# Carried attention blocks made whole, two address alignments in TensorE's program, and weight blocks split after the second network's input

## The reference

```python
# attention: q, k, v, f_logit are (4, 8, 768, 48)
f = 1 / (1 + exp(-f_logit))
for t in range(S):
    state = f[:, :, t, :, None] * state + einsum('bhd,bhe->bhde', k[:, :, t], v[:, :, t])
    y[:, :, t] = einsum('bhd,bhde->bhe', q[:, :, t], state)
x = y as (3072, 384)
# first network, d_ff = 1536
xn = x / sqrt(mean(x * x) + 1e-6) * rms_g
x = (silu(xn @ w_gate) * (xn @ w_val)) @ w_out
# second network, d_ff = 2048
h = x @ w_in
g = where(h >= 1, h, where(h <= -1, 0, (h + 1) ** 2 / 4))
out = g @ w_out
```

## Time and profile before

| | |
|---|---|
| median of 3 runs | 938.35 us (938.14 to 938.43) |
| profiled execution | 938.0 us |
| its span, first to last instruction | 936.2 us |
| granted TensorE clock | 1.000 |
| TensorE matmuls busy | 924.3 us, 99% of the span |
| TensorE weight loads busy | 784.0 us, 84% |
| VectorE busy | 555.2 us, 59% |
| ScalarE busy | 329.1 us, 35% |
| GpSimd busy | 15.7 us, 2% |

### The profile page before, as it was taken

One profiled execution on the slowest core, in us unless ns is written; L12 is line 12 of the kernel. 1 busy time (PEld: TensorE's weight loads), 2 busy tenths in 40 slices (PEclk: granted clock), 3 DMA queues, 4 the chain that ended last, 5 costly groups with the idle time before them and its releaser, 6 DMA issues.

```text
span 936.2 us, 18634 instructions
## 1 busy us (share of the span) xinstructions
PE 924.3 (99%) x7498; PEld 784.0 (84%) x7498; DVE 555.2 (59%) x971; ACT 329.1 (35%) x561; POOL 15.7 (2%) x35
## 2 busy tenths in 40 slices
PE   7999999999999999999999999999999999999998
PEld 4999999998888888888888788888888888888886
DVE  7987667756746675576545555445445445555453
ACT  4653233323223232332243433343334333333433
POOL 1000000000000000000000000000000000000000
PEclk9999999999999999999999999999999999999999
DMA  9622533532432341343222100000000000000000
GB/s 317 234 69 62 161 97 98 178 89 86 124 93 74 112 143 55 100 119 108 73 72 86 58 1 0 1 34 0 2 32 0 34 0 0 34 0 0 34 1 34
DMA packets 52129, 65.84 MB, mean 70 GB/s; under 512 B 14560, under 2 KB 42976, under 8 KB 52064
## 3 DMA queue, kind: packets, MB, share of 16 engines
q1 hardware_dynamic: 51920, 64.75, 22.1%
q10 hardware_dynamic: 144, 0.13, 0.0%
HBM read 51.43 MB, written 13.43 MB: 69 GB/s over the span
## 4 chain that ended last, share of the span: by engine, by line
PE 97%; issue 2%; DVE 1%; POOL 0%; ACT 0%; POOLq 0%; DVEq 0%; ACTq 0%
PE gate_ps L599 16%; PE val_ps L599 16%; PE acc L675 14%; PE gate_ps L663 10%; PE acc L621 10%; PE val_ps L663 10%; PE acc L679 7%; PE acc L625 5%; PE pair_ps L462 2%; PE y_ps L485 2%; PE y_ps L525 2%; PE pair_ps L514 1%; PE acc L690 0%; DVE low L1369 0%; PE pair_ps L445 0%
## 5 line engine op out<-in xcount | busy, mean ns | idle before, releaser
L950 ACT ACTIVATE raw<-raw,columns 128x512 f32<-128x512 f32 x96 | 69.4, 723 | 156.6 <-DVE raw L1392 156.6
L675 PE MATMUL acc<-high 128*128 128x512 f32 x282 | 109.9, 390 | 0.0
L675 PE MATMUL acc<-high,low 128*128 128x512 f32 x282 | 109.9, 390 | 0.0
L621 PE MATMUL acc<-high 128*128 128x512 f32 (+2 forms) x252 | 90.1, 362 | 0.0
L621 PE MATMUL acc<-high,low 128*128 128x512 f32 (+2 forms) x252 | 89.4, 359 | 0.0
L957 ACT ACTIVATE high<-qd 128x512 fp32r<-128x512 f32 x96 | 60.7, 632 | 73.1 <-DVE qd L1397 73.1
L679 PE MATMUL acc<-low,high 128*128 128x512 f32 x282 | 79.2, 389 | 0.0
L1392 DVE TENSOR_SCALAR raw<-val_ps 128x512 f32<-128x512 f32 x48 | 33.2, 691 | 77.5 <-PE val_ps L663 77.5
L1392 DVE TENSOR_SCALAR raw<-gate_ps 128x512 f32<-128x512 f32 x48 | 33.1, 689 | 62.7 <-PE gate_ps L663 62.7
L1329 DVE TENSOR_TENSOR low<-qd,high 128x512 fp32r<-128x512 f32 x96 | 65.7, 685 | 5.7 <-ACT high L957 5.1
L599 PE MATMUL gate_ps<-high 128*128 128x512 f32 (+2 forms) x252 | 66.3, 371 | 1.5 <-issue 0.6
(11 more groups left out here) (142 smaller groups left out, 1696.2 us busy)
## 6 DMA issues: line engine op xcount, KB each, us to landing
raw<-qkf_dram SPq DMA_DIRECT2D x22, 770.0 KB, 4.7
x_all<-wb_dram SPq DMA_DIRECT2D x12, 576.0 KB, 5.3
kd_turn_dram<-after SPq DMA_DIRECT2D x19, 256.0 KB, 3.0
kd<-kd_turn_dram SPq DMA_DIRECT2D x76, 64.0 KB, 2.5
v_sb<-v_dram SPq DMA_DIRECT2D x23, 192.0 KB, 2.9
v_early<-v_dram SPq DMA_DIRECT2D x23, 192.0 KB, 3.0
out_dram<-x_all SPq DMA_DIRECT2D x5, 768.0 KB, 3.8
x_turn_dram<-x_all SPq DMA_DIRECT2D x19, 192.0 KB, 1.8
```

The source lines that it names most:

```text
L621: pe.matmul(acc[:, m, 0:width(i)], wb_part(w, j, 2, m), h_hi[:, j % 2, 0:width(i)], start=(j == 0 and w is w_hi), stop=False)
L675: pe.matmul(acc[:, m, 0:N2], wc_part(w, j, 1, m), h2_hi[:, j % 2, :], start=(j == 0 and w is w_hi), stop=False)
L950: nc.scalar.activation(act2_buf[:, j % 2, :], act2_buf[:, j % 2, :], ACT.Square, bias=half_col[:, :], scale=0.5).then_inc(square_ready, 1)
```

## The change

Three things are edited.

The table `APART` and the parameter `state_done` go. Every carried block is issued whole, at its slot.

Two address alignments are put into TensorE's program, ahead of `project_out(1, 4)` and `project_out(3, 7)`.
In the last tile of the first network, VectorE's half of splitting weight blocks 13 and 14, which stood after j = 11, moves behind the low part of the second network's last input columns (line 1383) and of the last h, ahead of block 15. The edit is in VectorE's `gated_mlp`; ScalarE's order stays as it is.

```diff
-APART = {(2, 1): 2, (3, 0): 2, (3, 2): 2, (4, 0): 2, (5, 0): 2, (6, 1): 2}
+LINE = 256
+BEGINS = {(1, 5): 207, (3, 8): 254}
...
-                def attend(n, c, scores_next=False, state_done=False):
+                def attend(n, c, scores_next=False):
...
-                    if not state_done:
-                        attend_state(n, c)
+                    attend_state(n, c)
...
                 def attend_tile(i, slot, blocks):
                     for c, due in enumerate(blocks):
-                        sooner = APART.get((i, c), 0)
-                        if sooner and slot == due - sooner:
-                            attend_state(begin(i) + c, c)
                         if slot == due:
-                            attend(begin(i) + c, c, scores_next=c + 1 < len(blocks), state_done=sooner > 0)
+                            attend(begin(i) + c, c, scores_next=c + 1 < len(blocks))
...
                         value(i, j)
                         if following is not None:
                             attention(following, 3 * j + 1)
+                        if (i, j) in BEGINS:
+                            pe.addr_align(LINE, BEGINS[i, j])
                         if j > 0:
                             project_out(i, j - 1)
...
                         elif j == 1:
                             split_x2(0)
-                        else:
+                        elif j < JB - 1:
                             for jc in wc_due(j):
                                 split_wc(jc)
                     if following is None:
                         split_x2_last()
                     rest_h(i, JB - 1)
                     if following is None:
-                        for jc in wc_due(JB):
+                        for jc in (*wc_due(JB - 1), *wc_due(JB)):
                             split_wc(jc)
```

## The result

The changed kernel took 940.54 us (median of 12 executions, 938.85 to 942.22), the kernel before, run beside it, 938.24 us (12 executions, 937.54 to 940.41). The ratio is 1.0023, with a 95% interval of 1.0016 to 1.0030. That is slower by 0.23%, just above the 0.2% that the prediction took for the least difference to be told, where 935.0 us and faster were forecast. The profiled execution took 939.12 us, with a span of 937.4.

The account below looks back on a forecast made before the run. TensorE, with matmuls filling 99% of the span, was taken as the bound: 938.0 - 2.0 (whole blocks) - 1.3 (seam) + 0 (alignments) = 934.7, plus 0.35 for the median, 935.0 us; 8-in-10 range 934.3 to 938.3.

Parts of the forecast that it names:

- Part 1, whole blocks: On TensorE, issuing six split attention blocks whole saves switches between matmul sizes: 0.34 us each, 2.0 us together.
- Part 3, the seam: Between the networks, TensorE's wait for VectorE line 1383 ahead of `hidden(0, 0)` closes whole: 1.27 us.
- rival 4: The seam's gap comes back at the next wait, `hidden_out(0, 0)` behind `copy_x2`: up to 1.27 us, 936.3; chance 0.05.
- Part 2, the price of a pad: At the first alignment, 76 pads at 32 ns each take 2.4 us, hidden by the sequencer's lead: cost 0.
- The lead of the sequencer: TensorE's sequencer runs 2.95 us, 17 dense matmuls, ahead of the array, which hides pads up to that time.
- the limit of 39 ns: At the first alignment, 76 pads are free up to 2.95 / 76 = 39 ns each.
- the upper bound of 0.1 us: Spacing of TensorE's semaphore waits taken as a pad's highest price: 76 pads 7.6 us, 4.65 of them idle.
- Rival 2: Pads cost 0.1 us each, leaving 4.65 to 5.85 us idle before `project_out(1, 4)`: 939.7 to 940.9; chance 0.10.
- its threshold of 82 ns: Price per pad at the first alignment above which the change is a loss: (3.3 + 2.95) / 76.
- Part 2, what an edge costs: In whole blocks, each edge between 256-slot program pieces costs 0, with 0.25 us as the other end.
- Rival 3: Whole blocks lose 0.25 us each at piece edges: 938.3 with all 13, 936.0 with four; chance 0.11.
- The loop's new place: Pads move the second network's loop from slot 78 to 180, three pieces to four: cost 0.

Follow-up runs that it names:

- experiment 5: Changed kernel with five alignments instead of two, all jumped over by a branch, whole blocks placed far from late pieces: 935.32 us beside 938.04, ratio 0.9973.
- experiment 6: Kernel before with the seam mended and five jumped alignments, its six blocks still apart: 937.25 us beside 938.04, ratio 0.9997.
- experiment 1: Kernel before with only the weight blocks moved behind the second network's input: 936.64 us beside 937.75, ratio 0.9988.
- experiment 9: Changed kernel with four alignments, all jumped over by a branch instead of executing pads: 934.14 us beside 937.96, ratio 0.9959.
- experiment 2: Changed kernel without its two alignments, so whole blocks and mended seam but no pads: 937.72 us beside 937.75, ratio 1.0003.
- experiment 3: Changed kernel with the pads of both alignments jumped over by one branch, every instruction at the same slot: 937.05 us beside 937.75, ratio 0.9986.
- experiment 4: Changed kernel with a third alignment, splitting the 79 pads into executed stretches of 39 and 40: 937.27 us beside 937.75, ratio 0.9993.
- experiment 7: Kernel before with the first alignment alone, its 79 pads executed: 942.76 us beside 938.04, ratio 1.0048.
- experiment 11: Kernel of experiment 9, but with the first alignment's 79 pads executed instead of jumped: 938.41 us beside 937.96, ratio 1.0003.

## Why the prediction was wrong

**Part 1, whole blocks: right.** 0.34 and 0.35 us a block by the trace, 1.9 us for six by experiments 5 and 6 (forecast 2.0; by experiments 1 and 9 it would be 2.7, and neither is known better than by about 1.5 us). No semaphore takes it back.

**Part 3, the seam: right.** 1.1 us by experiment 1 (forecast 1.3), no gap at the next wait (rival 4).

**Part 2, the price of a pad: the step that failed.** The lead of the sequencer was right (2.95 us forecast, 3.1 measured), and so were the limit of 39 ns and the count (76, then 79). The value I took between the bounds was not. I chose 32 ns, the duration of a register operation, by the argument that a pad has neither register nor semaphore. The measured step is 73 ns, nearer to the upper bound of 0.1 us, and instead of the forecast 0 the array idled 2.7 us. The prediction itself said that the row doesn't show such an operation back to back, and a duration is not a spacing: the pads are recorded at 13 ns each. Here the lower bound from 288 array instructions in 2.90 us was no help either. Rival 2 had the mechanism, and its threshold of 82 ns was right for what it counted: at 73 ns the pads alone would have left a gain. That its 939.7 to 940.9 us takes in the measured 940.54 is luck: the pads' idle time is 2.7 us of it, not 4.65, and the rest came from terms that it did not have. The Trainium skill's floor of about 20 cycles per instruction (Runtime: NRT & Kernel Launch, Instruction fetch mechanics), for which I had worked out 17 ns, is lower than the pads' step in the trace by a factor of four. For array instructions it is too high: a whole block passes 288 of them in 2.90 us, 10 ns each.

**Part 2, what an edge costs: the second step that failed.** I read the earlier trace rows as a fixed loss of 0.25 us at an edge and, since the other blocks didn't show it, took 0. It was neither. In that trace the packet lands at 93.50, 1.25 us before the scores start at 94.75: a piece that came late by a little. The same scores take 0.95 us in the changed kernel, where the packet lands 2.65 us before them:

```profile
94.39 0.95 PE L463 MATMUL pair_ps<-qd,kd 64*64 64x128 f32 x32
```

Over all 13 traces the split is clean: where the packet lands 1.39 us or more before the scores (seven traces) they take 0.95 us, where it lands 1.25 us or less before (six) they take 1.20 to 1.79, the most in experiment 9. At the stalls of the 17 other places with a late piece the array goes on 1.30 to 1.59 us after the landing of the packet. An edge is free as long as its piece is in by then, and costs what it is late: 2.45 us at (4,1) and (6,2) of the changed kernel, where the forecast had 0. I had checked that no block *crosses* two edges; the two that stalled have their second edge 10 and 18 slots behind the block, and the array does the 256 small instructions ahead of it in 2.2 us, while the packet starts 2.1 to 3.8 us after the edge before it. (Edge times are estimates, from the array's times and the sequencer's lead of 37 instructions.) Rival 3 priced edges evenly at 0.25 us; the loss is 0 to 2 us in the few places where edges follow closely in time. The same section of the Trainium skill says that crossing an edge is "mostly hidden"; experiments 2 and 3 show where it isn't. The Trainium skill also warns there of a fetch stall behind a taken branch whose target isn't in the current two-page window. No run here shows where that window stood. On the sequencer two branches lasted 1.18 and 0.68 us (experiments 5 and 6, the target's piece just landed), the others 0.18 to 0.33; on the array the jumps, over 26 to 243 slots, left no issue entry.

**The loop's new place: right.** From 545 to 930 us PE is busy throughout in either trace.

**The clock: not in the prediction.** Among the 12 executions of the changed kernel, seven had a mean clock of 0.998 (940.25 to 942.22, median 940.61); the others' median is 939.12, still 0.9 us above the kernel before. A mean of 0.998 or less comes now and then without pads, too: in 2 of 68 executions of the kernel before, in 5 of 34 of experiments 1, 2 and 6. Experiments 3, 4, 5 and 9 had none below 0.999. The traces of experiments 7 and 11 show the fall right behind the idle time, and its 3.4 us at half clock are what makes a mean of 0.998; for the executions without a trace that place is inferred.

**The account.** Forecast 935.0. From experiment 9 to the changed kernel (ratios 0.9959 and, between its two measurements, 1.0022) are 5.9 us: the pads' idle time 2.7, the clock about 2 in half of the executions (counted as 1), and (4,1) and (6,2) together 2.1 to 3.0 in four profiles. These make 5.8 to 6.7; the spread of 935.55 to 937.76 in experiment 3, at full clock, may be what late pieces do from one execution to the next, which no trace here shows.

**Open:** what delays a packet. Behind a jump over an edge it starts 0.7 to 1.3 us after the end of the branch (experiments 5, 6, 9 and 11). In the whole blocks that stall it starts 2.1 to 3.8 us after the edge, and at (6,1) of experiment 2, which got through, 1.7 us. In block (2,0) it starts between 90.8 and 93.3 us in different traces at nearly the same pace of the array, and nothing else was moved by DMA from 88 to 92 in the traces of the changed kernel and of experiment 9. Open too is why the transposed x comes late near 168 us with five alignments.

## What to carry to other kernels

Count a no-operation on TensorE's sequencer at 73 ns and compare the stretch with the sequencer's lead at that place; where more pads are wanted, jump over them, which cost the sequencer one branch, 0.18 to 1.18 us, and the array nothing. A run of small matmuls uses up a piece of the program faster than the next one arrives, so place such runs by the time between two piece edges as the sequencer passes them, and look behind the run as well as inside it. And when an operation isn't in the trace, don't price it by the duration of a lone one of another kind: between bounds this far apart the forecast has to carry the upper one with real weight.

## What the runs showed of the hardware that I had not expected

- A pad is recorded as 13 ns and costs 73: sequencer rows show durations, only the distance of their starts shows the rate.
- From the landing of a late piece's packet to the first matmul out of it: 1.30 to 1.59 us, on top of 0.9 to 1.3 us for the packet.
- With 2.6 us of idle time in it, 20 of 35 executions of four kernels (the change twice, 7 and 11) had a mean clock of 0.998, against 2 of 68 of the kernel before at 0.998 or less. In the two traced ones the clock was at half, 1.2 GHz, for 3.4 us, from 1.4 and 0.2 us after work had resumed. With 8.5 us of idle time all four executions had a lower clock (in the traced one it fell within the idle time), with 0.7 us none of eleven.
- A taken branch over a skipped stretch of the program lasted 0.18 to 0.20 us within a piece, 0.28 to 0.33 into the next one, and 0.68 and 1.18 where that piece had just landed. With a lead of about 3 us none of them stopped the array.
